# Attention and two feed-forward layers on one core: value sums of both batches by one scheme, a bank of its own for tile 10, near scores of tile 0 ahead of the key maxima

## The reference

```python
k_sum = k.reshape(B, H, nb, block, D).max(axis=3)
v_sum = v.reshape(B, H, nb, block, D).mean(axis=3)
scores_l = scale * q @ k^T, masked to |i - j| < 16
scores_s = scale * q @ k_sum^T + log(block)
a = softmax(concat(scores_l, scores_s))
x = a @ concat(v, v_sum)                     # [1536, 512]
g = x @ w_gate; x = (silu(g) * (x @ w_val)) @ w_out      # d_ff 1536
h = x @ w_in;   x = g2(h) @ w_out2                       # d_ff 2048
```

## Time and profile before

| | us |
|---|---|
| median of 3 runs | 604.05 (602.78 to 607.47) |
| the profiled execution | 602.59 |
| its span, first to last instruction | 600.8 |
| TensorE matmul busy | 576.6 (96% of the span) |
| VectorE busy | 453.7 (76%) |
| ScalarE busy | 363.7 (61%) |
| GpSimd busy | 82.4 (14%) |

### The profile page before, as it was taken

The page is one execution under the profiler, slowest core; times in us unless marked ns, Lnnn a source line. Parts: engine busy times, 40 slices in busy tenths (PEclk is TensorE's granted clock), DMA queues, the critical chain, the costliest instruction groups (busy, mean ns, idle before and its releaser), DMA issues.

```text
span 600.8 us, 10664 instructions
## 1 busy us (share of the span) xinstructions
PE 576.6 (96%) x3960; PEld 537.5 (89%) x3960; DVE 453.7 (76%) x902; ACT 363.7 (61%) x734; POOL 82.4 (14%) x80
## 2 busy tenths in 40 slices
PE   3888899999999999999999999999999999999997
PEld 2767799999899999999999999998778999988886
DVE  5669688777586568888686668998997579979833
ACT  4986888889654465555545456665565456655522
POOL 3940331233300002332200000000000000000000
PEclk9999999999999999999999999999999999999999
DMA  9996634252022112223221112321121423012112
GB/s 332 231 315 170 162 123 126 78 194 71 21 73 67 35 36 71 71 78 130 73 71 56 51 35 71 123 88 53 53 69 37 141 71 122 2 39 78 60 52 106
DMA packets 31535, 57.64 MB, mean 96 GB/s; under 512 B 3196, under 2 KB 6012, under 8 KB 31484
## 3 DMA queue, kind: packets, MB, share of 16 engines
q1 hardware_dynamic: 31484, 56.96, 29.8%
HBM read 52.23 MB, written 3.15 MB: 92 GB/s over the span
## 4 chain that ended last, share of the span: by engine, by line
PE 85%; DVE 8%; ACT 3%; issue 2%; DMA 1%; POOL 0%; POOLq 0%; SPq 0%; DVEq 0%; ACTq 0%
PE ps L615 47%; PE ps L761 18%; PE ps L727 15%; PE ps L605 2%; PE ps L585 2%; DVE hid_lo L1272 1%; PE ps L578 1%; DMA k_raw<-k_t_dram 1%; DVE rel L1278 1%; DVE h L1281 1%; PE ps L564 1%; DVE x_lo L1205 1%; ACT prob_s L877 1%; DVE k_sum L1143 1%; DVE t_late L1198 1%
## 5 line engine op out<-in xcount | busy, mean ns | idle before, releaser
L615 PE MATMUL ps<-x_hi,w_hi 128*128 128x384 f32 x560 | 190.4, 340 | 3.2 <-DVE part L1249 1.3
L615 PE MATMUL ps<-x_lo,w_hi 128*128 128x384 f32 x560 | 187.5, 335 | 0.0
L615 PE MATMUL ps<-x_hi,w_lo 128*128 128x384 f32 x560 | 187.4, 335 | 0.0
L615 PEld LDWEIGHTS ps<-x_hi,w_hi 128*128 128x128 f32 x560 | 105.1, 188 | 8.0 <-issue 2.6
L615 PEld LDWEIGHTS ps<-x_hi,w_lo 128*128 128x128 f32 x560 | 105.2, 188 | 0.1
L615 PEld LDWEIGHTS ps<-x_lo,w_hi 128*128 128x128 f32 x560 | 105.1, 188 | 0.0
L997 ACT ACTIVATE wout_hi<-wout_raw 128x512 fp32r<-128x512 f32 x56 | 35.3, 631 | 95.1 <-PE ps L761 51.9
L761 PE MATMUL ps<-wout_hi,hid_hi 128*128 128x512 f32 x192 | 74.8, 390 | 0.7 <-DVE wout_lo L1266 0.7
L761 PE MATMUL ps<-wout_hi,hid_lo 128*128 128x512 f32 x192 | 75.2, 391 | 0.1
L761 PE MATMUL ps<-wout_lo,hid_hi 128*128 128x512 f32 x192 | 74.8, 390 | 0.0
L1266 DVE TENSOR_TENSOR wout_lo<-wout_raw,wout_hi 128x512 fp32r<-128x512 f32 x56 | 38.6, 689 | 42.3 <-ACT wout_hi L997 42.0
(11 more groups left out here) (122 smaller groups left out, 898.1 us busy)
## 6 DMA issues: line engine op xcount, KB each, us to landing
w_raw<-w_dram SPq DMA_DIRECT2D x80, 256.0 KB, 3.0
wout_raw<-w_dram SPq DMA_DIRECT2D x56, 256.0 KB, 2.6
out_dram<-y_out SPq DMA_DIRECT2D x12, 256.0 KB, 2.1
v_s<-v_rows_dram SPq DMA_DIRECT2D x6, 384.0 KB, 8.8
v_a<-v_rows_dram SPq DMA_DIRECT2D x6, 384.0 KB, 3.6
v_tok_a<-v_rows_dram SPq DMA_DIRECT2D x3, 512.0 KB, 7.8
k_raw_b<-k_t_dram SPq DMA_DIRECT2D x3, 512.0 KB, 4.6
v_tok_b<-v_rows_dram SPq DMA_DIRECT2D x3, 512.0 KB, 8.3
```

What stands on the lines that cost most here:

```text
L615: last = nc.tensor.matmul(dst, lhs, rhs, start=start and kk == 0 and i == 0, stop=kk == 1 and i == 2, skip_group_check=not start)
```

## The change

1. Batch 0's keys come in four pieces (14, 14, 12, 8 of 48 sub-blocks), and the load of tile 0's queries stands ahead of the last piece. `key_maxima` splits a piece where it crosses the two halves of `k_sum`, so there are five reductions where there were three.
2. Tile 0's near scores wait for the first keys and the queries only; its far scores come behind both near groups and wait for the maxima.
3. `value_sums(b)` does both batches by the first batch's scheme. ScalarE copies the second batch's sums to `v_sum` with four instructions of 32 x 128, and one DMA takes the place of four. It stands ahead of the loads of tiles 14 and 15.
4. Tile 10's transposes go to bank AT1, so they do not wait for the copy of tile 9, and stand ahead of tile 8's value product. ScalarE's and VectorE's programs are written in another order around it: the copy of pair 3 stands later, `w_hi_a(1)` before the copy of pair 5; the second batch's first two key maxima stand before the two `x_lo`, the sums of x in another order, and `c22(0)` ahead of `w_lo_b(1)` and the mask of tile 12.

```diff
+KSPLIT = (0, 14, 28, 40, 48)
+KPIECES = len(KSPLIT) - 1
-        trans_ps = quads(X1)
+        def first_trans_ps(s):
+            return quads(AT1 if s == LAST_A - 2 else X1)
             def place_late_sums():
                 sp.wait_ge(v_sum_ready, 2)
                 sp.wait_ge(trans_done, LAST_A)
-                for j in range(4):
...
-                    sp.dma_start(v_a[row:row + n, :, y * (DM // 2):(y + 1) * (DM // 2)], part_of).then_inc(v_late_sums, 16)
+                sp.dma_start(v_a[WIN:], v_sum[WIN:].unsqueeze(1).to_broadcast([P - WIN, 4, DM])).then_inc(v_late_sums, 16)
-            for c in range(3):
+            for c in range(KPIECES - 1):
                 load_k_raw(0, c)
             load_q(0)
+            load_k_raw(0, KPIECES - 1)
             load_late(6)
             load_w(3)
+            place_late_sums()
             load_late(7)
-            place_late_sums()
-            def late_value_sums():
+            def value_sums(b):
+                if b:
+                    pe.wait_ge(masked_ready, LAST_A - 1)
+                    pe.wait_ge(prob_t_ready, LAST_A)
...
                 if s == 0:
-                    pe.wait_ge(k_sum_ready, 3)
+                    pe.wait_ge(k_raw_loaded[0][0], 16)
...
+                order = ((0, near), (1, near), (0, far), (1, far)) if s == 0 else ((0, near), (0, far), (1, near), (1, far))
+                for i, (x, (k, lo, hi)) in enumerate(order):
+                    if s == 0 and i == 2:
+                        pe.wait_ge(k_sum_ready, KPIECES)
...
+                elif s == LAST_A - 2:
+                    pe.wait_ge(masked_ready, s + 1)
+                elif s == LAST_A - 1:
+                    pe.wait_ge(prob_t_ready, s - 1)
             first_transposes(LAST_A - 3)
+            first_transposes(LAST_A - 2)
             first_values(8)
-            first_transposes(LAST_A - 2)
+            first_transposes(LAST_A - 1)
             first_values(9)
-            first_transposes(LAST_A - 1)
             def copy_late_sums():
                 act.wait_ge(v_sum_done, 2)
-                nc.scalar.activation(v_part[:], v_sum_ps[1][:, 0:DM // 2], ACT.Copy).then_inc(v_sum_ready, 1)
+                for done in v_first_sums:
+                    act.wait_ge(done, 16)
+                for j in range(4):
+                    last = nc.scalar.activation(v_sum[WIN:, j * QUARTER:(j + 1) * QUARTER],
+                                                v_sum_ps[1][BLOCK * j:BLOCK * j + BLOCK, 0:QUARTER], ACT.Copy)
+                last.then_inc(v_sum_ready, 1)
-            first_copy_out(3)
-            copy_trans(LAST_A - 3, trans_ps)
-            x_part_hi(0, X_B11)
-            copy_trans(LAST_A - 2, trans_ps)
+            copy_trans(LAST_A - 3, first_trans_ps(LAST_A - 3))
+            x_part_hi(0, X_B11)
+            copy_trans(LAST_A - 2, first_trans_ps(LAST_A - 2))
+            first_copy_out(3)
             x_part_hi(0, X_B21)
...
+            w_hi_a(1)
             first_copy_out(5)
-            w_hi_a(1)
...
+                if k == 0 and m == X_B21:
+                    dve.wait_ge(attn_done, 9)
...
+                    if late and r == 1:
+                        w_lo_b(u)
+                        mask_scores(LAST_A)
```

More of the change, by code:

```diff
@@ L245, in build @@
         filled = sem("filled")
-        k_raw_loaded = [[sem(f"k_raw_loaded{b}{c}") for c in range(3)] for b in range(B)]
+        k_raw_loaded = [[sem(f"k_raw_loaded{b}{c}") for c in range(KPIECES if b == 0 else 3)] for b in range(B)]
         sel_ready = sem("sel_ready")
@@ L556, in first_scores @@
                 if s == 0:
-                    pe.wait_ge(k_sum_ready, 3)
-                keys = k_raw[:, QT // SUB * s:QT // SUB * s + WSUBS], k_sum[:, 0]
-                for x in range(2):
-                    for k, lo, hi in ((keys[0], 0, WIN), (keys[1], WIN, COLS)):
-                        for half, row in ((0, 0), (1, 1), (1, 0), (0, 1)):
-                            a = pair_at(2 * row + x, half)
-                            rows = slice(row * D, row * D + D)
-                            last = nc.tensor.matmul(dst[half * QT:half * QT + QT, row, x * COLS + lo:x * COLS + hi],
-                                                    q[rows, r, a], k[rows, :, a], start=True, stop=True)
+                    pe.wait_ge(k_raw_loaded[0][0], 16)
+                near = k_raw[:, QT // SUB * s:QT // SUB * s + WSUBS], 0, WIN
+                far = k_sum[:, 0], WIN, COLS
+                order = ((0, near), (1, near), (0, far), (1, far)) if s == 0 else ((0, near), (0, far), (1, near), (1, far))
+                for i, (x, (k, lo, hi)) in enumerate(order):
+                    if s == 0 and i == 2:
+                        pe.wait_ge(k_sum_ready, KPIECES)
+                    for half, row in ((0, 0), (1, 1), (1, 0), (0, 1)):
+                        a = pair_at(2 * row + x, half)
+                        rows = slice(row * D, row * D + D)
+                        last = nc.tensor.matmul(dst[half * QT:half * QT + QT, row, x * COLS + lo:x * COLS + hi],
+                                                q[rows, r, a], k[rows, :, a], start=True, stop=True)
                 last.then_inc(scores_done, 1)
@@ L1141, in key_maxima @@
                 dve.wait_ge(k_raw_loaded[b][c], 16)
[L1142 to L1143 removed]
+                n0, n1, src = key_blocks(b, c)
+                for i in range(n0 // SUB, (n1 - 1) // SUB + 1):
+                    lo, hi = max(n0, SUB * i), min(n1, SUB * i + SUB)
+                    last = nc.vector.tensor_reduce(k_sum[:, b, i, :, lo - SUB * i:hi - SUB * i], src[:, :, lo - n0:hi - n0],
+                                                   AX.XY, ALU.max)
+                last.then_inc(k_sum_ready, 1)
             def place_v_sum():
@@ L1305, in _ @@
             dve.wait_ge(pads_ready, 1)
-            for c in range(3):
+            for c in range(KPIECES):
                 key_maxima(0, c)
```

78 lines of the change are left out of this document (32 added, 46 removed).

## The result

The changed kernel is a little faster: median 602.77 us of 22 runs (599.98 to 604.49), against 604.43 us of 22 runs of before (601.64 to 607.47). The ratio is 0.9965, its 95% interval 0.9949 to 0.9982, so the gain is 2.1 us (1.1 to 3.1); the two medians alone differ by 1.66. Forecast were 599.2 us, and 595.8 to 602.6 for the range; the time stands just outside it, at half the gain that I had summed. The profiled execution of after took 601.27 us (span 599.3), against 602.59 us (600.8).

What follows compares the result with a forecast made beforehand. Before 69 us each stage is bounded by another engine; after it TensorE runs without notable waits. Gains 0.6 + 0 + 2.1 + 1.45 = 4.15 us off the profiled 602.59 give 598.4, adjusted to 599.2 us; range 595.8 to 602.6.

Steps and rivals of the forecast that it cites:

- head: Tile 0: near scores run hidden under the last key maximum, so its mask starts earlier; gain 0.6 us, bounds 0.2 to 0.8.
- tile 10's bank: Before the first product: tile 11's transposes still need GpSimd's last normalisation, so gain 0, bounds 0 to 0.5 us.
- late sums: Tile 12's value product: one early transfer removes its 1.96 us wait, 0.5 given back; gain 1.45 us, bounds 0 to 1.96.
- Middle: First product to p7(1): VectorE's new order brings the last x_lo and c22(0) earlier; gain 2.1 us, bounds 1.2 to 2.5.
- rival A: The unnamed wait before tile 12's value product is no transfer: the 1.45 us goes, 600.7 us; chance 0.13.
- `p1_copy(2)` on ScalarE is next: Late stage, behind tile 13's exponentials: this copy makes p6(2) wait, giving back 0.5 us.
- ScalarE's four copies: Second batch's value sums: four 32x128 copies take 1.0 us, bounded by 1.54, and x_hi of T3 and T4 stays in time.
- The base: Start of the sum: profiled 602.59 us less the gain, plus half its 1.5 us distance to the three-run median, 604.05.
- Rival C: VectorE, first phase: key maximum (1,0) waits for a late key load and delays everything; 605.0 us; chance 0.03.
- Rival D: Near scores start no earlier as q_a lands at 7.8, and ScalarE takes back VectorE's gain; 602.0 us; chance 0.07.
- Rival B: Head, bank, middle and late stages all pay more, 5.8 us together; 597.6 us; chance 0.17.
- all is decided before 69 us: Whole kernel: TensorE runs without notable waits after 69 us, so only earlier time can change.

Runs made afterwards that it cites:

- after_again: The changed kernel run once more, unedited, for a second profile: 602.21 us, ratio 0.9983 to the kernel before.
- late4: The changed kernel with the late sums as before (12 matmuls, one copy, four transfers behind the next pair's loads): 602.44 us, ratio 0.9961 to before.
- midonly: The kernel before with only the new order on VectorE and ScalarE and tile 10's transposes in their own bank: 601.62 us, ratio 0.9976 to before.
- before_3: The kernel before, unedited, run again for its third profile: 606.64 us.
- before_6: The kernel before, unedited, run again for its sixth profile: 606.71 us.
- nohead: The changed kernel with three key pieces ahead of the queries and tile 0's scores waiting for all maxima, as before: 602.31 us, ratio 0.9978 to before.
- near3: The changed kernel with three key pieces and the queries behind them, tile 0's near scores still early: 601.74 us, ratio 0.9979 to before.
- oldmid: The changed kernel with VectorE's order as before, from the first x_lo to tile 12's mask: 604.57 us, ratio 1.001 to before.
- warm2: near3 with 15 spare matmuls ahead of tile 0 and 5 behind tile 2's scores, results thrown away: 602.89 us, ratio 0.9969 to before.
- after_3: The changed kernel, unedited, run again for its third profile: 601.39 us.
- near3_warm: near3 with 22 spare matmuls on TensorE ahead of tile 0, results thrown away: 602.74 us, ratio 0.9988 to before.
- lateonly: The kernel before with only the new late sums, tile 10's bank and ScalarE's order, VectorE's order as before: 603.9 us, ratio 1.0011 to before.
- relief: near3 with SP waiting for the sixth tile before loading w_raw(1) and the value slabs of tiles 8 to 11: 605.49 us, ratio 1.0021 to before.
- before_2: The kernel before, unedited, run again for its second profile: 607.71 us.
- before_4: The kernel before, unedited, run again for its fourth profile: 606.63 us.

## Why the prediction was wrong, step by step

The sign, "within 1%" and the main mechanism were right; the size was not. Means over the profiles of before (six) and of after (three) give, stage by stage: head 0.29, stage A 1.74 (1.34 with after_again, where `v_tok_b` landed late), B 0.35, and tile 10's bank 0.25, together 2.6 us (2.2), within the measured 1.1 to 3.1. The steps that failed are the late sums, by 1.1 us, and the head, by 0.3.

**Middle, 2.1 forecast, 1.84 measured in the pair, up to p7(1): right.** Counted from the first product, p3(0) was to start at 13.48 and started at 13.80 (before 15.69), p7(1) at 16.46 and 16.70 (before 18.54). Of what is missing, 0.27 us stand at the last `x_lo`, forecast at 10.21 and started at 10.48, since ScalarE's `x_hi` comes late (0.17 us idle at 52.56). In late4, without the four copies, it started at 10.23. Undoing this order gives the whole difference back (1.001, partly by the 0.64 us above); keeping it without head and late sums leaves 0.9976, whose interval still takes in 1. This order is the change's gain as far as the stages tell; the measured ratios of the other parts alone hold no effect that their intervals could show.

**Late sums, 1.45 forecast, 0.35 measured: the step that failed.** "So this wait goes in full" was right, and rival A most likely wrong: none of the ten profiles with the one early transfer has the wait, five of the eight with four late ones do. What failed is the size, a single execution's 1.79 us taken as the kernel's own. In six profiles of before it was 1.79, 1.11, 0.29, nothing, nothing, 0.66. B was 9.19 and 8.50 in the first two and 7.86 to 8.05 in the other four; the changed kernel stands at 7.87 to 7.90. In the pair itself the stage gave 1.32, near the 1.45. The distance was not what varied: from the issue of the fourth transfer to where the value product could have started are 5.9 to 6.0 us in all six. What varied is how long the queue took: the load of `v_a` issued just ahead of the four landed 9.9, 9.6, 8.6, 8.4, 8.3 and 9.1 us after its issue, and the longer this took the longer was the wait (the trace has no landing for each of the four themselves). Why it took longer in some executions stays open.

A second part of this step failed too: at 1.0 us for ScalarE's copies, `x_hi` of T4 was to be ready before VectorE asks, so they were put at nothing. They cost 0.27 us of stage A (17.88 in after, 17.61 in late4 and 17.60 in midonly, the two with the new order and one copy). From the first product to tile 13's transposes late4 and midonly take 25.50 and 25.49 us and after 25.75. So beside the new order the late sums gave nothing that these profiles show. That `p1_copy(2)` on ScalarE is next was right: forecast 0.5, seen 0.43. By that, a wait of up to half a microsecond costs little or nothing (B is 7.86 in before_3 with 0.29, and 8.05 in before_6 with 0.66).

**Head, 0.6 forecast, 0.12 in the pair, 0.29 in the mean: the second step that failed.** "The last key piece lands at 7.81 and `q_a` at 7.1" was wrong. `q_a` landed at 2.12 + 5.5 = 7.62 and the piece at 2.59 + 5.7 = 8.29 (its maximum started at 8.36). These two lines stand in the table of DMA issues, with size and time to landing:
```profile
k_raw<-k_t_dram SPq DMA_DIRECT2D x1, 288.0 KB, 5.7
q_a<-q_t_dram SPq DMA_DIRECT2D x1, 256.0 KB, 5.5
```
The same bytes in five transfers took half a microsecond longer than in four in this pair, and 0.3 us over all profiles (last landing 8.34 in the mean of the five with five transfers, 8.04 in that of the thirteen with four). The last maximum ended at 9.05, not 8.55. I had this as a lower bound (0.2), and should have leaned on it: I reckoned bytes only, with nothing for the transfer itself. The maxima came out as reckoned, 0.69 us for 512 elements against 0.68. That the 0.29 us at the mask reach the first product is not shown.

**Tile 10's bank, 0 forecast, 0.25 measured.** From the end of tile 11's exponentials to the first product takes 4.06 or 4.07 us with it (after, after_again, nohead, near3, late4, oldmid, midonly, warm2), and 4.31 or 4.32 in five profiles of before. In the other five profiles (before_3, after_3, near3_warm, lateonly, relief) TensorE ran at a mean granted clock of 0.50 to 0.64 over the 4.3 us ahead of the first product, and the stretch took 4.62 to 6.87. My argument went by GpSimd's normalisation alone. Bank and ScalarE's new order are together in all these kernels, so no run says which of them gives the 0.25.

**ScalarE's four copies, 1.0 taken, 1.11 measured.** By the budget of the Trainium skill (ScalarE: Activation LUTs, Rules for kernel authors) they would take an estimated 1.6 us; the row disagrees: each copy took 0.27 us, 0.28 from start to start. Even so they were late for VectorE, as said above.

**The base.** I took 602.59 us, the profiled execution, as nearly typical, and added 0.8, which is 603.4; the median of before is 604.43. So 1.0 us of the 3.6 by which the forecast missed is the base, and the other 2.5 the gain (4.15, against 1.66 between the medians). The profile's first product, at 40.49, is the earliest of all 18; the other five of before stand at 42.63 to 46.36. So I subtracted a gain from a lucky first 40 us. (The later profiles are no better guide to it: the mean span is 603.8 us in six of before and 599.6 in three of after, twice the measured gain apart.) Two things set that stretch: the pace of TensorE, and the unnamed stall. Kernels with and without the change show both, and nothing here ties either to the change. In the pair they cost after 0.47 + 0.96 + 0.60 = 2.0 us: from mask 0 to the value sums 5.38 against 4.91, the sums 2.48 against 1.52, the stall 1.28 against 0.68. Less 0.12 and 0.25 won, that is the 1.6 us by which its first product is late.

Rival C was not seen: no profile has an engine that waits for a batch 1 key load behind 36 us. Rival D's time, 602.0, is the nearest to what was measured, but by luck: its `q_a` half was right (7.6 and not 7.1), while the middle order was not taken back. Rival B's size did not come. That all is decided before 69 us was right in every profile.

## What to carry to other kernels

Before a wait becomes a term of a sum, look for it in several executions of the same kernel: one that ends with a transfer's landing may be 1.8 us in one and nothing in the next, at the same distance from issue to reader, while the stretch set by engine order (VectorE's instruction behind work that nobody needs yet) was 19.70 or 19.71 us in five of six profiles of before. Undo each part of a change by itself: the late sums saved a wait in one stage and put 0.27 us on ScalarE in another. Take the base from the runs' median and not from one profile, and check first how usual its early stretch is. Splitting a load to get something earlier has a price of its own, here 0.3 to 0.5 us on the last piece.

## What was not expected of the hardware

**TensorE has two paces at the same granted clock reading.** Between 10 and 19 us its rows run at half pace (48 records of the value sums, 24 matmuls, in 2.48 to 2.79 us, four of transposes in 1.09) or at full pace (1.52 and 0.63), while the granted clock reads 1.00 in that stretch in all profiles but near3_warm's. The sums ran at full pace in 4 of 18 profiles (before, near3, midonly, warm2). Later falls do show in the column: 0.50, the 1.2 GHz level, behind an idle stretch of 2 us in near3_warm, above, and behind the unnamed stall in before_2, before_3, before_4, before_6, nohead, oldmid, relief and warm2 (1.70 to 3.48 us), though not in near3 (1.83) and late4 (1.98). In before_2 it reads 0.66 in the 5 us behind the 2.63 us stall:
```profile
33.00:38.00 5.00, 4.82 (x77) 3.92 (x80) 1.85 (x11) 3.05 (x13) 3.59 (x5) 0.66 0.68 167
```
The Trainium skill (TensorE: Matmul & The Clock Gate, Part 1) says that "the default state is throttled, and activity releases the throttle". The spare matmuls ahead of tile 0 agree with it: in near3_warm their records stand 0.21 us apart up to 7.7 us and 0.11 us apart from there on, in warm2 the pace rises at 5.6 us, and the granted clock reads 1.00 on both sides. The falls behind idle stretches agree too. (So what I had written ahead of warm2, the lower pace to 10 us, misread near3_warm.) Why one execution is fast from 11.9 us and the next of the same kernel from 17 us or later was not settled.

**A stall at a fixed count of instructions.** In 15 of 18 profiles it stands before the last matmul record of tile 5's value product, 0.4 to 3.5 us long, with no releaser; after_3 has none. Ahead of it the trace records 961 instructions on TensorE (471 matmuls, 472 weight loads, 18 semaphore instructions), the same in all 15. With 22 matmuls put ahead in near3_warm it stood behind 1217, 256 more; with 20 spare ones in warm2 behind 961 again, at another place of the program, and another of its stalls behind 450, 511 fewer (its third, behind 733, does not fit). So it goes by the count of instructions, in steps of about 256, and not by the data. An almost empty DMA queue did not remove it. A fetch of instructions fits: the Trainium skill (Advanced Engine Details and Errata, ISA Cache) gives the instruction cache lines of 16 KB with 256 instructions each, and the steps agree with that. But no run shows the fetch itself, and what sets its length, which decides several microseconds between executions, stays open. It is not from the change: the kernels with all, some or none of its parts have it.
